# Fused attention and expert layer: DMA issues moved between queues and two pieces of VectorE work reordered

## The chip, the cores and the metric

The kernel runs on one core of one Trainium2 chip. The metric is the device time of one execution in microseconds (us); lower is better. The engines are named PE (TensorE), ACT (ScalarE), DVE (VectorE), POOL (GpSimd) and SP (SyncE).

## The reference

Squared-relu attention in fp32, over 8 batches of 3072 tokens with 256 columns of u and v and 64 columns of z, and then a mixture of 8 experts:

```
scores = (z @ z.T) / S                       # S = 3072, per batch
x      = u * (maximum(scores, 0)**2 @ v)     # rows of all batches, one after the other
logits = x @ w_gate;  e = argmax(logits);  gate = softmax(logits)[e]
# the first `capacity` (768) tokens of each expert are kept, in order; others give 0
out[i] = gate[i] * (maximum(x[i] @ w1[e], 0) @ w2[e])   if i is kept, else 0
```

Once all experts are full, later tokens can't change the output.

## The kernel before

**Arithmetic.** All products run in fp16 with the operands split in a high and a low half, so that each product is three matmuls (high x high, high x low, low x high).

**Groups and pairs.** The attention stage works on groups of 384 queries (three tiles of 128), numbered n = 0, 1, 2, ...; eight groups make a batch (g = n & 7). Group 0 is written out ("peeled"), the others are one loop body per engine (`attention_loop`, L232). A group has 12 steps, one for each pair of key chunks (2 x 128 keys), numbered c = 0 to 11. Work on a pair passes PE (`scores`, L678), ACT (`do_relu` L495, then `do_square` L502), DVE (`do_hi` L1013 casts the fp32 weights to fp16, `do_lo` L1022 takes the rest) and again PE (`weigh`, L731, 18 matmuls). PE does the scores in bursts of three pairs, at c = 0, 3, 6 and 9, each burst three pairs ahead; the burst at c = 9 makes the first three pairs of the next group. ACT runs three pairs ahead of `weigh`, DVE two.

**A finished group.** At c = 11 DVE multiplies the sums with u (`gate_x`, L1056, into ubuf). In the next group, at c = 0, ACT takes row sums of absolute values (l1, L524), DVE makes a power-of-two row scale from them (rscale L1107, rowfac L1110), ACT writes the high halves of the scaled rows (rows_hi, L542) and DVE the low halves (rows_lo, L1117). For each of the three tiles, SP then issues a transposing DMA (xT, L282). PE multiplies xT with the gate weights after tile 1 of c = 3 (logits, L791) and counts the tokens of each expert after tile 1 of c = 4 (counts, L800 and L804). DVE's route at c = 3 takes both: maximum, below, one-hot (up to L1174), then positions from the counts (L1182 to L1189), the flag (`full`, L1191), the softmax sum from ACT's exp (L563; L1195 to L1198) and the slots (L1200 to L1202). POOL scatters the rows to `disp` by slot (L411).

**The end of the stage.** The flag says whether all experts are full. Every engine waits for it and loads it into a register after c = 5 (DVE after c = 4), and does the rest of the group only if the flag allows it (`both_parts`, L248, `load_end`, L241). With these inputs that happens in group n = 18. Then the expert stage follows, 8 experts in halves of 384 rows.

**Queries and keys.** Group n's scores read its 384 queries from q_now (pairs 3 to 11) or q_next (pairs 0 to 2, made in group n - 1), and the first keys of the next batch from k_next. POOL fills these from zP and zQ by DMA within its part of the loop, behind its scatters, when the scores that read the old contents are done (L385 to L398, L424 to L434). PE waits for them at c = 0 and c = 9 (L760 to L769). At c = 5 it also waits, ahead of the flag, for the keys and for the relu that frees the last banks of scores of the group (L762 to L765); `scores` then leaves its own wait for relu_done out in pairs 9 to 11.

**Order of work.** Each engine runs its own instructions in the order in which they are written; semaphores order the engines among each other. `wait_apart` (L218) is a wait on a value in a register, with an increment of a semaphore (`passed`) behind it.

Of the kernel before, what the change touches and what calls it, by code (L numbers as in the profile page):

```python
# [15 lines left out]
I32 = mybir.dt.int32  # L16
# [6 lines left out]
P = 128  # L23
# [23 lines left out]
def relu2_attention_moe(nc, u, v, z, w_gate, w1, w2, out, disp, capacity):  # L47
# [13 lines left out]
    with ExitStack() as ctx:  # L61
# [67 lines left out]
        least = sb("least", [P, 1], F32)  # L129
        full = sb("full", [1, 1], I32)  # L130
        dues = sb("dues", [1, RING], I32)
# [109 lines left out]
        def load_end(eng, n, end):  # L241

            if isinstance(n, int):
                return
            wait_apart(eng, s["flag_ready"], n)
            eng.reg_load(end, full[0:1, 0:1])

# [129 lines left out]
        def _(pool):  # L377
# [3 lines left out]
            pool.partition_all_reduce(amx[:, 1:2], mx[:, 1:2], P, RMAX).then_inc(s["amx0"], 1)  # L381

            def queries(to, m, loaded):

                for key in ("khi_ready", "klo_ready"):  # L385
                    wait_apart(pool, s[key], (m & 126) + 2)
                for q, z16 in zip(to, (zP, zQ)):
                    pool.dma_start(q[:, :], z16[:, bass.ds((m & 15) * GROUP, GROUP)]).then_inc(s[loaded], 16)

            def first_keys(m):  # L390

                for k, z16 in zip(k_next, (zP, zQ)):
                    pool.dma_start(k[:, :], z16[:, bass.ds((m & 8) * (S // 8), SLICE * P)]
                                   ).then_inc(s["loaded_k_next"], 16)

            queries(q_now, 1, "loaded_q_now")
            queries(q_next, 2, "loaded_q_next")
            first_keys(0)  # L398
            pool.wait_ge(s["gmx_ready"], 1)
            pool.partition_all_reduce(gamx[:, :], gmx[:, :], P, RMAX).then_inc(s["gamx_ready"], 1)  # L400

            def body(n, end):
# [21 lines left out]
                def rest():  # L424
                    wait_apart(pool, s["scores_ready"], n * PAIRS + PAIRS)
                    queries(q_now, n + 1, "loaded_q_now")
                    wait_apart(pool, s["scattered"], n * 48)
                    pool.sem_inc(s["row_free"], 1)
                    only_if(pool, g == 3, reduce_maxes)
                    only_if(pool, n == 7, lambda: all_w(0))  # L430
                    only_if(pool, n == 12, lambda: all_w(1))
                    wait_apart(pool, s["scores_ready"], n * PAIRS + PAIRS + BURST)
                    queries(q_next, n + 2, "loaded_q_next")
                    only_if(pool, g == 6, lambda: first_keys(n + 2))  # L434
                only_if(pool, pool.snap(end) > 0, rest)
# [26 lines left out]
        def _(act):  # L462
# [50 lines left out]
            v_hi(UNIT, UNIT)  # L513

            def body(n, end):
                g = n & 7
                peeled = isinstance(n, int)
                K0 = n * PAIRS
                def part(start, stop):
                    for c in range(start, stop):  # L520
# [5 lines left out]
                        if peeled:  # L526
                            if c == 0 or c % BURST:
                                do_relu(K0 + c + 2, c + 2)
                            do_square(K0 + c + 2, c + 2)
                            if c % BURST == 2:  # L530
                                do_relu(K0 + c + 3, c + 3)
                            if c == PAIRS - 1:
                                do_square(K0 + c + 3, c + 3)
                        elif c % BURST == 0:
                            do_relu(K0 + c + 3, c + 3)
                        elif c % BURST == 1:
                            do_relu(K0 + c + 3, c + 3)
                            do_relu(K0 + c + 4, c + 4)
                        if not peeled and c == ROWS_HI_AT:
                            act.wait_ge(s["rscale_ready"], n)  # L540
# [46 lines left out]
                def first_groups(c):  # L587
# [15 lines left out]
                    for q, (group, at) in enumerate(W_HI_IN):  # L603
                        if c == at:
                            only_if(act, n == group, lambda: split_w_hi(0, 0, q))
                both_parts(act, n, end, part)

# [52 lines left out]
        def _(pe):  # L660
# [17 lines left out]
            def scores(K, n, c, par):  # L678


                if not isinstance(K, int):
                    if par is None or c < PAIRS - BURST:
                        wait_apart(pe, s["relu_done"], K - BURST + 1)
                elif K >= BURST:
                    pe.wait_ge(s["relu_done"], K - BURST + 1)
# [40 lines left out]
            def body(n, end, par):  # L726
# [18 lines left out]
                def part(start, stop):  # L745
                    for c in range(start, stop):
                        def burst():
                            first = c + BURST
                            if first < PAIRS:
                                if peeled:  # L750
                                    wait_keys(2 * (first // BURST) + 2, False)
                                for k in range(first, first + BURST):
                                    scores(K0 + k, n, k, par)
# [6 lines left out]
                        if not peeled and c == 0:  # L760
                            wait_apart(pe, s["loaded_q_now"], n * 32)
                        if not peeled and c == END_AT:  # L762

                            wait_keys((n & 120) + 8)
                            wait_apart(pe, s["relu_done"], K0 + PAIRS - BURST)  # L765
                        if not peeled and c == PAIRS - BURST:
# [145 lines left out]
        def _(dve):  # L912
# [161 lines left out]
            def body(n, end):  # L1074
# [21 lines left out]
                def part(start, stop):  # L1096
                    for c in range(start, stop):
# [13 lines left out]
                        if c == PAIRS - 1:  # L1111

                            gate_x(n + 1)
                        if not peeled and c == ROWS_LO_AT:
                            for t in range(TILES):
# [4 lines left out]
                                ins.then_inc(s["rows_lo"], 1)  # L1120
                        do_hi(K0 + c + 2, c + 2, n)
                        do_lo(K0 + c + 2, c + 2)
                        if not peeled and c == DUE_AT:
# [38 lines left out]
                        if not peeled and c == ROUTE_AT[0]:  # L1162
# [12 lines left out]
                                              ).then_inc(s["onehot_ready"], 1)  # L1175
                        if not peeled and c == ROUTE_AT[1]:
                            dve.wait_ge(s["counts_ready"], n)
                            counts = small_counts[:, 0:TILES * E].rearrange("p (t e) -> p t e", t=TILES)

                            def over_tiles(x):  # L1180
# [9 lines left out]
                                                           in1=posf[:, :, :], op0=ALU.mult, op1=ALU.add))  # L1190
                            dve.tensor_scalar(full[0:1, 0:1], least[0:1, :],  # L1191
                                              0.0, float(NG + 1), ALU.is_lt, ALU.mult
                                              ).then_inc(s["flag_ready"], 1)
                            dve.wait_ge(s["exp_ready"], n)
                            route(dve.tensor_reduce(exsum[:, :], ex[:, :, :], AX.X, ALU.add))  # L1195
                            route(dve.scalar_tensor_tensor(out=exsum[:, :], in0=exsum[:, :], scalar=1e-9, in1=rscale[:, :],
                                                           op0=ALU.add, op1=ALU.mult))
                            dve.reciprocal(xrow[:, :, D:D + 1].rearrange("p t a -> p (t a)"), exsum[:, :]  # L1198
                                           ).then_inc(s["slot_ready"], 1)
                            route(dve.tensor_tensor(posf[:, :, :], posf[:, :, :], onehot[:, 0:TILES, :], ALU.mult))  # L1200
# [179 lines left out]
EXP_AT = 4  # L1380
ROUTE_AT = (3, 3)
END_AT = 5
# [12 lines left out]
VLO_AT = (7, 8)  # L1395
ROUTE_STEPS = 2 + 4 + 3 + 2

# [42 lines left out]
```

## Time and profile before

| | |
|---|---|
| median of 3 runs | 860.57 us (860.52 to 860.78) |
| the profiled execution, its own time | 860.57 us |
| its span, first to last instruction | 858.7 us |
| mean granted clock of TensorE | 0.999 of full speed |
| attention stage | to about 602 us |
| expert stage | from there to the end |
| queues | SP and ACT: hardware DMA queue, POOL: software DMA queue |

The profile is of one execution. Times are microseconds from the start of the span. A timeline row gives start, duration, engine, line, operation, output<-input and in brackets the idle time of the engine ahead of it and whose work ended it. The ends of matmuls are modelled: they are pipelined, and neighbours overlap in the record. Register, branch, semaphore and DMA-issuing instructions are not counted as busy.

### The profile page before, as it was taken

How to read it: one execution, taken by the hardware profiler on the slowest of the kernel's cores; microseconds unless marked ns; L12 is line 12 of the kernel's file. 1: busy time of each engine (PE TensorE's matmuls, PEld its weight loads, DVE VectorE, ACT ScalarE, POOL GpSimd, SP SyncE). 2: the span in 40 equal slices, each digit the busy share in tenths (PEclk: the TensorE clock that was granted, in tenths of full speed). 3: DMA queues.
4: the chain of work that ended last, by engine and by line, in shares of the span. 5: the costliest groups of instructions: out<-in, count | busy, mean ns of one | idle time of the engine just before them, and what ended most of it. 6: DMA issues, size and time to landing. Idle time of an engine off the chain costs nothing.

```text
span 858.7 us, 24366 instructions
## 1 busy us (share of the span) xinstructions
PE 835.7 (97%) x7714; PEld 649.0 (76%) x7714; DVE 631.2 (74%) x1360; ACT 561.4 (65%) x873; POOL 167.5 (20%) x198
## 2 busy tenths in 40 slices
PE   6999999999999999999999999999999999999997
PEld 5777777777777777877877877777677777777776
DVE  7977877889889888887888888787555655565521
ACT  7978777768768768776878778578434434435422
POOL 2003202202302211211211320220121221211212
PEclk9999999999999999999999999999999999999999
DMA  8923353343323723313314324722616325415201
GB/s 292 395 72 112 105 171 121 116 155 126 132 58 123 280 82 124 127 49 116 128 49 134 128 62 152 270 71 64 156 46 167 128 62 153 147 43 153 55 18 37
DMA packets 108118, 106.90 MB, mean 124 GB/s; under 512 B 68397, under 2 KB 94202, under 8 KB 107072
## 3 DMA queue, kind: packets, MB, share of 16 engines
q1 hardware_dynamic: 99360, 85.71, 32.2%
q0 software_dynamic: 8736, 20.90, 6.8%
q8 instruction: 13, 0.21, 0.1%
q14 instruction: 9, 0.07, 0.0%
HBM read 40.03 MB, written 44.93 MB: 99 GB/s over the span
## 4 chain that ended last, share of the span: by engine, by line
PE 73%; DVE 12%; issue 9%; DVEq 3%; ACT 2%; POOL 0%; ACTq 0%; POOLq 0%
PE Sc L862 15%; PE O L737 12%; PE O L741 11%; PE O L739 11%; PE Sc L703 9%; DVE attn_hi L1019 4%; PE O L885 3%; PE O L887 3%; PE O L889 3%; DVE attn_lo L1025 2%; ACT xrow L542 2%; PE Sc L885 2%; PE Sc L887 2%; PE Sc L889 2%; DVE ubuf L1066 1%
## 5 line engine op out<-in xcount | busy, mean ns | idle before, releaser
L737 PE MATMUL O<-vS,attn_hi 128*128 128x256 f16 x1332 | 363.9, 273 | 9.9 <-DVE attn_lo L1025 8.5
L741 PE MATMUL O<-vS,attn_lo 128*128 128x256 f16 x1332 | 363.0, 273 | 0.0
L739 PE MATMUL O<-vS,attn_hi 128*128 128x256 f16 x1332 | 363.0, 273 | 0.0
L499 ACT ACTIVATE attn<-Sc 128x768 f32<-128x768 f32 x225 | 172.7, 799 | 100.8 <-DVE attn_lo L1025 63.6
L1025 DVE TENSOR_TENSOR attn_lo<-attn,attn_hi 128x768 f16<-128x768 f32 x223 | 213.7, 958 | 7.7
L504 ACT ACTIVATE attn<-attn 128x768 f32<-128x768 f32 x225 | 185.2, 840 | 3.6 <-ACT xT L474 1.4
L737 PEld LDWEIGHTS O<-vS,attn_hi 128*128 128x128 f16 x1332 | 129.9, 98 | 52.3 <-DVE attn_lo L1025 20.8
L741 PEld LDWEIGHTS O<-vS,attn_lo 128*128 128x128 f16 x1332 | 130.2, 98 | 15.1
L1329 DVE SCALAR_TENSOR_TENSOR rawv<-Sc,rawv 128x768 f16<-128x768 f32 x63 | 60.1, 956 | 110.0 <-ACT rawv L622 64.4
L739 PEld LDWEIGHTS O<-vS,attn_hi 128*128 128x128 f16 x1332 | 130.3, 98 | 13.8
L411 POOL DMA_INDIRECT disp<-xrow,slot x54 | 67.9, 1258 | 366.8 <-DVE slot L1201 355.9
L1019 DVE CAST attn_hi<-attn 128x768 f16<-128x768 f32 x223 | 124.1, 556 | 17.4 <-ACT attn L504 12.7
L622 ACT ACTIVATE rawv<-Sc 128x768 f16<-128x768 f32 x63 | 51.0, 810 | 100.8 <-PE Sc L862 92.8
L703 PE MATMUL Sc<-q_now,zP 64*128 64x384 f16 x477 | 86.7, 324 | 0.1
L703 PE MATMUL Sc<-q_now,zQ 64*128 64x384 f16 x477 | 86.4, 324 | 0.0
L862 PE MATMUL Sc<-vS,w1h 128*128 128x384 f16 x384 | 78.1, 326 | 0.0
L885 PE MATMUL O<-w2s,rawv 128*128 128x256 f16 x256 | 69.8, 273 | 0.0
L889 PE MATMUL O<-w2s,rawv 128*128 128x256 f16 x256 | 69.8, 273 | 0.0
L887 PE MATMUL O<-w2s,rawv 128*128 128x256 f16 x256 | 69.8, 273 | 0.0
L451 POOL DMA_INDIRECT out<-attn,vS x48 | 47.0, 980 | 113.0 <-ACT attn L634 99.8
L703 PEld LDWEIGHTS Sc<-q_now,zP 64*128 64x128 f16 x477 | 40.8, 94 | 25.0 <-issue 11.3
L862 PEld LDWEIGHTS Sc<-vS,w1h 128*128 128x128 f16 x384 | 37.6, 98 | 21.0
(167 smaller groups left out, 1031.5 us busy)
## 6 DMA issues: line engine op xcount, KB each, us to landing
out<-empty SPq DMA_DIRECT2D x16, 1536.0 KB, 5.9
wraw<-in_moe_w SPq DMA_DIRECT2D x16, 1024.0 KB
rawv<-in_v SPq DMA_DIRECT2D x14, 768.0 KB, 7.6
ubuf<-in_u SPq DMA_DIRECT2D x19, 384.0 KB, 3.2
disp<-vS SPq DMA_DIRECT2D x8, 774.0 KB, 11.5
rawz<-in_z SPq DMA_DIRECT2D x3, 768.0 KB
q_now<-zP POOLq DMA_DIRECT2D x18, 96.0 KB, 2.0
q_now<-zQ POOLq DMA_DIRECT2D x18, 96.0 KB, 1.9
```

Of the source, the lines that this page charges most:

```text
L499: act.activation(attn[:, c % BUFS, :, :], Sp[:, score_banks(c), 0:GROUP], ACT.Relu).then_inc(s["relu_done"], 1)
L504: act.activation(attn[:, c % BUFS, :, :], attn[:, c % BUFS, :, :], ACT.Square, scale=ROOT_C).then_inc(s["square_done"], 1)
L703: ins = nc.tensor.matmul(Sp[:, 2 * (c % BURST) + r, 0:GROUP], keys[r], queries[r], start=at == 0, stop=at == len(terms) - 1)
L737: nc.tensor.matmul(o_part(t), hi, v[:, 0:D], start=c == 0 and j == 0 and t % 2 == 0, stop=False, skip_group_check=True)
L739: nc.tensor.matmul(o_part(t), hi, v[:, D:2 * D], start=False, stop=False, skip_group_check=True)
L741: ins = nc.tensor.matmul(o_part(t), lo, v[:, 0:D], start=False, stop=c == PAIRS - 1 and j == 1, skip_group_check=True)
L862: ins = nc.tensor.matmul(Sp[:, 2 * (p % 2) + fi, 0:GROUP], w[par][:, m, f * P:(f + 1) * P], xt[k][:, x + m, :], start=(at == 0), stop=(at ...
L885: nc.tensor.matmul(y_part(t), hi, w2s[:, par, f, 0:D], start=f == 0, stop=False, skip_group_check=True)
L887: nc.tensor.matmul(y_part(t), hi, w2s[:, par, f, D:2 * D], start=False, stop=False, skip_group_check=True)
L889: ins = nc.tensor.matmul(y_part(t), lo, w2s[:, par, f, 0:D], start=False, stop=f == FC - 1, skip_group_check=True)
L1019: dve.tensor_copy(attn_hi[:, b, :, :].rearrange("p j n -> p (j n)"), attn[:, b, :, :].rearrange("p j n -> p (j n)")).then_inc(s["hi_done"], 1)
L1025: dve.tensor_tensor(attn_lo[:, b, :, :], attn[:, b, :, :], attn_hi[:, b, :, :], ALU.subtract).then_inc(s["lo_done"], 1)
```

## The change

Five edits:

1. The DMAs for q_now, q_next and k_next go from POOL's queue to ACT's. ACT issues q_now for the next group at c = 7 (`Q_NOW_AT`) and q_next at c = 10 (`Q_NEXT_AT`), each behind the relus that wait for the scores concerned, and waits for all of them at the end of its group. POOL keeps the scatters and the reductions; its wait for the scatters and the increment of row_free now stand outside the part that depends on the flag.
2. At c = 0 DVE does `do_hi` and `do_lo` (of pair 2) ahead of rows_lo and no longer behind them.
3. In the route, DVE does the softmax sum ahead of the wait for the counts. Since rscale is not folded in any more, the division becomes a reciprocal and a multiplication with rinv: four small instructions in place of three.
4. The flag becomes a ring of four (`ends`), read by an address worked out from n.
5. PE's waits for the keys and for relu_done move from c = 5 to the burst at c = 6, pair by pair, and PE waits for counts_read at c = 6.

```diff
-            eng.reg_load(end, full[0:1, 0:1])
+            eng.reg_load(end, ends[0:1, bass.ds((n - 1) & (RING - 1), 1)])
...
# POOL
-            queries(q_now, 1, "loaded_q_now")
-            queries(q_next, 2, "loaded_q_next")
-            first_keys(0)
...
                 def rest():
-                    wait_apart(pool, s["scores_ready"], n * PAIRS + PAIRS)
-                    queries(q_now, n + 1, "loaded_q_now")
-                    wait_apart(pool, s["scattered"], n * 48)
-                    pool.sem_inc(s["row_free"], 1)
                     only_if(pool, g == 3, reduce_maxes)
                     only_if(pool, n == 7, lambda: all_w(0))
                     only_if(pool, n == 12, lambda: all_w(1))
-                    wait_apart(pool, s["scores_ready"], n * PAIRS + PAIRS + BURST)
-                    queries(q_next, n + 2, "loaded_q_next")
-                    only_if(pool, g == 6, lambda: first_keys(n + 2))
+                wait_apart(pool, s["scattered"], n * 48)
+                pool.sem_inc(s["row_free"], 1)
...
# ACT
+            def queries(to, m, loaded):
+                for q, z16 in zip(to, (zP, zQ)):
+                    act.dma_start(q[:, :], z16[:, bass.ds((m & 15) * GROUP, GROUP)]).then_inc(s[loaded], 16)
+            def first_keys(m):
+                for k, z16 in zip(k_next, (zP, zQ)):
+                    act.dma_start(k[:, :], z16[:, bass.ds((m & 8) * (S // 8), SLICE * P)]
+                                  ).then_inc(s["loaded_k_next"], 16)
+            def keys_split(m):
+                for key in ("khi_ready", "klo_ready"):
+                    wait_apart(act, s[key], (m & 126) + 2)
...
                         elif c % BURST == 1:
                             do_relu(K0 + c + 3, c + 3)
                             do_relu(K0 + c + 4, c + 4)
+                        if c == Q_NOW_AT:
+                            keys_split(n + 1)
+                            queries(q_now, n + 1, "loaded_q_now")
+                            if peeled:
+                                first_keys(0)
+                        if c == Q_NEXT_AT:
+                            keys_split(n + 2)
+                            queries(q_next, n + 2, "loaded_q_next")
+                            if not peeled:
+                                only_if(act, g == 6, lambda: first_keys(n + 2))
...
-                both_parts(act, n, end, part)
+                def part_and_copies(start, stop):
+                    part(start, stop)
+                    if stop == PAIRS:
+                        wait_apart(act, s["loaded_q_now"], n * 32 + 32)
+                        wait_apart(act, s["loaded_q_next"], n * 32 + 32)
+                        wait_apart(act, s["loaded_k_next"], ((n + 2) & 120) * 4 + 32)
+                both_parts(act, n, end, part_and_copies)
...
# PE
-                    if par is None or c < PAIRS - BURST:
-                        wait_apart(pe, s["relu_done"], K - BURST + 1)
+                    wait_apart(pe, s["relu_done"], K - BURST + 1)
...
+                                elif first == PAIRS - BURST:
+                                    wait_keys((n & 120) + 8)
...
-                        if not peeled and c == END_AT:
-                            wait_keys((n & 120) + 8)
-                            wait_apart(pe, s["relu_done"], K0 + PAIRS - BURST)
+                        if not peeled and c == PAIRS - 2 * BURST:
+                            wait_apart(pe, s["counts_read"], n)
...
# DVE
+                        do_hi(K0 + c + 2, c + 2, n)
+                        do_lo(K0 + c + 2, c + 2)
                         if not peeled and c == ROWS_LO_AT:
                             for t in range(TILES):
...
-                        do_hi(K0 + c + 2, c + 2, n)
-                        do_lo(K0 + c + 2, c + 2)
...
                         if not peeled and c == ROUTE_AT[1]:
+                            dve.wait_ge(s["exp_ready"], n)
+                            route(dve.tensor_reduce(exsum[:, :], ex[:, :, :], AX.X, ALU.add))
+                            route(dve.tensor_scalar(exsum[:, :], exsum[:, :], 1e-9, None, ALU.add))
+                            route(dve.reciprocal(exsum[:, :], exsum[:, :]))
+                            dve.tensor_tensor(xrow[:, :, D:D + 1].rearrange("p t a -> p (t a)"), exsum[:, :], rinv[:, :],
+                                              ALU.mult).then_inc(s["slot_ready"], 1)
+                        if not peeled and c == ROUTE_AT[2]:
                             dve.wait_ge(s["counts_ready"], n)
...
-                            dve.tensor_scalar(full[0:1, 0:1], least[0:1, :],
+                            dve.tensor_scalar(ends[0:1, bass.ds((n - 1) & (RING - 1), 1)], least[0:1, :],
                                               0.0, float(NG + 1), ALU.is_lt, ALU.mult
                                               ).then_inc(s["flag_ready"], 1)
-                            dve.wait_ge(s["exp_ready"], n)
-                            route(dve.tensor_reduce(exsum[:, :], ex[:, :, :], AX.X, ALU.add))
-                            route(dve.scalar_tensor_tensor(out=exsum[:, :], in0=exsum[:, :], scalar=1e-9, in1=rscale[:, :],
-                                                           op0=ALU.add, op1=ALU.mult))
-                            dve.reciprocal(xrow[:, :, D:D + 1].rearrange("p t a -> p (t a)"), exsum[:, :]
-                                           ).then_inc(s["slot_ready"], 1)
...
-ROUTE_AT = (3, 3)
+Q_NOW_AT = 7
+Q_NEXT_AT = 10
+ROUTE_AT = (3, 3, 3)
```

## Rows read from the trace of the kernel before

**Rows 1.** Page, part 1: busy us, share of the span, instructions.

```profile
PE 835.7 (97%) x7714; PEld 649.0 (76%) x7714; DVE 631.2 (74%) x1360; ACT 561.4 (65%) x873; POOL 167.5 (20%) x198
```

**Rows 2.** Waits of PE: who waited for whom, us in total, times, longest.

```profile
PE O L737 <- DVE attn_lo L1025: 8.5, 18, 1.2
```

**Rows 3.** Timeline of PE, group 9: start, us, [idle before <-releaser].

```profile
302.69 0.33 PE L703 MATMUL Sc<-q_now,zP 64*128 64x384 f16 x1
...
308.68 0.28 PE L737 MATMUL O<-vS,attn_hi 128*128 128x256 f16 x1 [0.32 <-DVE attn_lo L1025]
...
310.75 0.33 PE L703 MATMUL Sc<-q_now,zP 64*128 64x384 f16 x1
...
313.64 0.45 PE L791 MATMUL Sc<-wgs,xT 128*128 128x16 f16 x12
...
318.72 0.33 PE L703 MATMUL Sc<-q_now,zP 64*128 64x384 f16 x1
...
326.29 1.64 PE L703 MATMUL Sc<-q_next,k_next 64*128 64x384 f16 x18
```

**Rows 4.** Timeline of DVE, group 9.

```profile
305.13 0.17 DVE L1107 TENSOR_SCALAR rscale<-rinv 128x3 int32<-128x3 int32 x1
...
305.87 1.28 DVE L1117 SCALAR_TENSOR_TENSOR xrow<-ubuf,rscale,xrow 128x256 f16<-128x256 f32 x3 [0.45 <-ACT xrow L542]
...
307.66 0.96 DVE L1025 TENSOR_TENSOR attn_lo<-attn,attn_hi 128x768 f16<-128x768 f32 x1
...
316.19 0.16 DVE L1182 TENSOR_TENSOR base<-base,Sc 128x8 f32<-128x8 f32 x1 [0.66 <-PE Sc L804]
...
317.06 0.14 DVE L1191 TENSOR_SCALAR full<-least 1x1 int32<-1x1 f32 x1
...
318.55 0.96 DVE L1025 TENSOR_TENSOR attn_lo<-attn,attn_hi 128x768 f16<-128x768 f32 x1
319.43 0.56 DVE L1019 CAST attn_hi<-attn 128x768 f16<-128x768 f32 x1
```

**Rows 5.** Timeline of ACT, group 9.

```profile
302.92 0.42 ACT L524 ACTIVATE xrow<-ubuf 128x256 f16<-128x256 f32 x1 [1.41 <-DVE ubuf L1066]
...
315.32 0.22 ACT L563 ACTIVATE ex<-logit 128x24 f32<-128x24 f32 x1
```

**Rows 6.** Timelines of SP and ACT; DMA issues (KB each, median us to landing).

```profile
306.46 3.97 SPq L282 DMA_TRANSPOSE xT<-xrow  x3
...
xT<-xrow SPq DMA_TRANSPOSE x54, 2.4
...
0.71 0.88 SPq L261 DMA_DIRECT2D rawz<-in_z  x2
...
rawz<-in_z SPq DMA_DIRECT2D x2, 384.0 KB, 3.5
...
3.96 1.79 ACT L468 ACTIVATE attn<-rawz 128x768 bf16<-128x768 f32 x2 [1.75 <-DMA rawz<-in_z]
```

**Rows 7.** DMA issues on POOL (groups by line: busy us, mean ns) and SP.

```profile
L388 POOL DMA_DIRECT2D q_now<-zP x18 | 12.2, 680 | 0.0
...
310.70 0.37 SPq L283 DMA_DIRECT2D ubuf<-in_u  x1
```

**Rows 8.** Timelines of DVE and PE, group 8.

```profile
273.96 0.17 DVE L1107 TENSOR_SCALAR rscale<-rinv 128x3 int32<-128x3 int32 x1
...
277.50 0.28 PE L737 MATMUL O<-vS,attn_hi 128*128 128x256 f16 x1 [1.18 <-DVE attn_lo L1025]
...
282.46 0.45 PE L791 MATMUL Sc<-wgs,xT 128*128 128x16 f16 x12
```

**Rows 9.** Timelines of DVE and PE, group 11.

```profile
390.07 0.55 DVE L1255 TENSOR_REDUCE mx<-Sc 128x1 f32<-128x384 f32 x1
...
391.44 1.64 PE L703 MATMUL Sc<-q_next,k_next 64*128 64x384 f16 x18 [1.55 <-DVE mx L1255]
```

**Rows 10.** Timeline of PE, the close of group 18.

```profile
601.99 0.49 PE L819 MATMUL O<-vS,attn_hi 128*128 128x256 f16 x3
```

More of the change, by code:

```diff
@@ L129, in relu2_attention_moe @@
         least = sb("least", [P, 1], F32)
-        full = sb("full", [1, 1], I32)
+        ends = sb("ends", [1, RING], I32)
         dues = sb("dues", [1, RING], I32)
@@ L381, in _ @@
             pool.partition_all_reduce(amx[:, 1:2], mx[:, 1:2], P, RMAX).then_inc(s["amx0"], 1)
[L383 to L394, printed above, removed]
-            queries(q_now, 1, "loaded_q_now")
-            queries(q_next, 2, "loaded_q_next")
-            first_keys(0)
             pool.wait_ge(s["gmx_ready"], 1)
@@ L1395 @@
 VLO_AT = (7, 8)
-ROUTE_STEPS = 2 + 4 + 3 + 2
+ROUTE_STEPS = 2 + 2 + 2 + 4 + 2
 _INS = ['u', 'v', 'z', 'moe_w_gate', 'moe_w1', 'moe_w2']
```

## The prediction

> **What bounds the kernel now.** I read the engines' shares first: TensorE (PE) is busy for 97% of the span [rows 1]. So time can only come from the places where PE stands still. The waits of PE say where [rows 2]: nearly all its idle time is one kind, 18 waits for attn_lo of VectorE (DVE), 8.5 us in the model of the trace, one in each attention group n = 1 to 18. The expert stage (from 602 us) has none worth naming and the change doesn't touch it. Then I read PE's timeline over group n = 9 [rows 3]. Score bursts start at 302.69, 310.75, 318.72 and 326.29: pitches of 8.06, 7.97 and 7.57 us. 7.57 is three pairs of chunks with nothing between. The second pitch has the logits and counts matmuls in it (0.40, real work). The first is 0.49 too long, and that is the wait at 308.68, which the trace prints as 0.32. It understates each such wait by 0.17, since the modelled end of a matmul overlaps the next one. So the loss is 8.5 + 18 x 0.17 = 11.6 us, 1.3% of the run, and no more than that can be had here, but for one wait in group 11 (below).
>
> **The stall and its release (do_hi/do_lo ahead of rows_lo).** In group 9, DVE has written rowfac and then waits 0.45 us for ACT's xrow, from 305.42 to 305.87, does the three rows_lo (1.28), and only then the hi and lo of pair 2, whose lo runs from 307.66 to 308.62; PE starts at 308.68 [rows 3, 4]. The square of that pair belongs to the group before, so its data lie ready. The two take 1.47 together (308.62 less the end of rows_lo, 305.87 + 1.28 = 307.15). Put first, hi starts at 305.42 and lo ends at 306.89. PE wants it at 308.68 - 0.49 = 308.19: 1.3 us to spare. In group 8, where the wait was longest (1.18 printed, 1.35 real), rscale starts at 273.96, two small steps (0.29, from the same steps in group 9: 305.42 less 305.13) and 1.47 bring lo's end to 275.72, and PE wants it at 277.50 - 1.35 = 276.15 [rows 4, 8]. Still early. All 18 waits go: **-11.6 us**.
>
> What is late next: pair 3's hi starts when rows_lo end, 306.89 + 1.28 = 308.2, lo ends 309.7, and PE wants pair 3 after the burst and pair 2, at 310.26 + 1.6 = 311.9. Fine.
>
> The price is that rows_lo move back by the 1.47 less the 0.45 of waiting: 1.02. Behind them is SyncE: three transposes, issued back to back in 3.97 us from 306.46, 2.4 us to landing [rows 6]. The last starts at about 306.46 + 2.71 = 309.17 and lands at 311.6; PE wants it at 313.64, a slack of 2.0. After the change it lands at 312.6 and PE comes at 313.15: slack 0.55. In group 8 PE comes 1.35 earlier: 282.46 - 1.35 = 281.11 [rows 8]; the same chain counted from rscale (309.17 + 2.4 + 1.02 - 305.13 = 7.4) gives 281.4, less 0.35 for the shorter route (next part) 281.05. That is level. Five groups have waits of the long kind, 5 to 8 and 10 (the longest, 8, is shown), and are near this; bounds for them 0 to 0.4 us each. I take **+0.3 us** in all.
>
> **The route on DVE.** Now DVE waits 0.66 us for the counts [rows 4] and later does three steps on exsum. Those go into the wait, as four (the division is now a reciprocal and a multiply). They need exp: ACT's exp ends at 315.54 [rows 5], onehot at 316.19 - 0.66 = 315.53, so the new wait for exp is 0.05 at most. Four small steps of 0.15 (six steps from 316.19 to 317.06) to 0.2 each are 0.6 to 0.8: the flag comes between 0.1 earlier and 0.2 later against PE than before, and the end of the route is some 0.35 earlier (0.66 less one more step, less the exp wait). It gains only where DVE is late afterwards: PE's wait of 1.55 for mx in group 11 [rows 9], **-0.35 us**.
>
> **Queries and keys issued by ACT and no longer by POOL.** Per group four plain DMAs, two at pair 7 and two at pair 10, and two more in groups 0, 6 and 14. No row shows one on ACT. POOL's take 0.68 us to issue (by software), SyncE's plain load 0.37 [rows 7]. Bounds 0 and 0.68, I take 0.4, nearest to SyncE's: 1.6 us on ACT per group. Behind them in ACT's queue stand square 10 and squares 13 and 14. ACT is busy for 65% of the span and idles 1.41 ahead of a group's l1 [rows 1, 5]; these squares are one pair ahead of DVE, so I expect that nothing reaches PE. POOL loses four waits and the DMAs and only has the scatter left: no gain, nobody waited for it. The new waits of ACT at the end of a group, for q_now, q_next and k_next: the last is issued some 2.5 us before ACT's idle time ends and takes 2.4 by the old queue, so it hides in the 1.41. Where a weight split stands at pair 10 (groups 8, 9) up to 0.8 us of it may push l1, and then the transposes, once or twice. Group 0 keeps ACT full and takes six issues. **+0.3 us** (0 to 1.5).
>
> **PE's own queue at pair 6.** The waits for relu_done and for the keys move from pair 5, ahead of the flag's load and branch, to the burst behind them, and counts_read and a ring address are added. The semaphores themselves are all set early: relu 8 stands ahead of the exp of 315.32 in ACT's queue and the counts are read before the flag of 317.06, against a burst at 318.72. What may cost is the queue's walk: flag written by 317.20, burst at 318.72, so 1.52 us [rows 3, 4], about 1.35 to 1.5 after the change. Load and branch take at most 0.88 (DVE does both, with two more waits, between lo 6 at 318.55 and hi 7 at 319.43 without idle), and on PE at the last group's turn they show no gap at all [rows 4, 10]. In group 11, mx ends at 390.62 and the burst starts at 391.44: 0.82 for leaving a branch and about five waits with their increments [rows 9]. Five waits more and the address are then 0.3 to 0.8. Sum 0.9 to 1.6 against 1.35 to 1.5: bounds 0 to 0.25 us in each of 17 groups, 0 to 4 us. I take **0**, since most of 0.88 is probably DVE's two other waits.
>
> This needs PE's queue to run ahead of its array by over a microsecond, and in the last group it runs ahead by at least the load and branch. The Trainium skill (Advanced Engine Details and Errata, Engine Queue Depths) gives TensorE a queue of 64 entries and VectorE and ScalarE one of 8. By that rule PE has some 30 matmuls in hand, and the walk is hidden as far as the flag allows: 0 us; with a short queue it would be the upper bound. The gapless close of the last group agrees with the rule as far as it goes.
>
> **Sum.** The profiled run took 860.57 us (span 858.7 and 1.9 around it), which is also the median. 860.57 - 11.6 - 0.35 + 0.3 + 0.3 = **849.2 us**.
>
> **Rivals.**
> A. *The queue walk at pair 6 shows.* For it: everything moved there sits behind a load and a branch. Against: now the pitch up to that burst is 7.57 and the 0.40 of real work, so load and branch cost nothing there [rows 3]. 17 x 0.15 to 0.45 = 2.5 to 7.5 us: about **854 us**.
> B. *The transposes become the wait (slower).* If a landing time counts from the issue's end and not from its start, the last one lands 1.2 later: 313.8 in group 9, and PE, due at 313.15, waits 0.7. 13 groups of 0.7 and 5 of about 1.2 are 15.1 us: **864 us**. It decides from a landing 0.55 us later than I reckon. Against: the first loads were issued at 0.71, take 3.5 to landing and ACT starts on the first at 3.96, which fits only a count from the start [rows 6].
> C. *A DMA issue holds ACT for far longer,* say until it lands (2 us). Then squares come 4 us late where they are at most some 2 ahead of need, and PE stands 2 us in each group: 849.2 + 2 x 18 = **885 us**. Against: POOL and SyncE issue in 0.7 and 0.4 [rows 7].
> D. *The stall comes back one step later,* half of it, because DVE, busy for 74% of the span [rows 1] and fuller in the groups that also split keys, values or weights, can't follow a faster PE: **855 us**. Against: the long waits are in 5 groups only, and the change frees 0.8 us of DVE per group (0.45 and 0.35). If instead nothing at all is gained, 860.6.
>
> **Chances.** Forecast 0.68, A 0.14, B 0.07, C 0.03, D 0.08 (of it 0.04 with no gain). This kernel's change is told from none at about 0.2%, 1.7 us. Faster: 0.68 + 0.14 + 0.04 = 0.86; same 0.04; slower 0.10. The forecast's own range is 847.5 to 851.5; with A and the better half of D the range is 847 to 857, which leaves out some 0.17.
>
> **What would show it.** Right: PE's waits for attn_lo gone (under 1 us in all), the first pitch of a group 7.6 and the group's period 30.7 us; DVE without the 0.45 before xrow and the 0.66 before base; the last transpose landing about 0.5 before the logits; ACT's DMA issues at 0.3 to 0.5 each. A: the gap ahead of the pair-6 burst over 0.21. B: PE or DVE waiting for xT at the logits, a second pitch over 7.97. C: ACT idle after its DMAs and the squares late. D: waits for attn_lo left in groups 5 to 8.

## The result and the profile after

The changed kernel takes 868.49 us (median of 4 runs, 867.05 to 870.21) against 860.67 before: the ratio is 1.0091, 95% interval 1.007 to 1.0111, so it is **slower by 0.9%**. I had forecast 849.2. The profiled execution took 866.55 us (span 864.8).

First the waits of PE in the changed kernel (who waited for whom, us in total, times, longest), to be read against [rows 2]:

```profile
PE Sc L712 <- issue: 8.5, 19, 0.7
...
PE Sc L800 <- DMA xT<-xrow: 3.8, 6, 0.7
PE O L746 <- DVE attn_lo L1034: 2.2, 4, 0.7
```

The wait for attn_lo (8.5 us before) is down to 2.2, and two new ones stand in its place: score bursts (L712) late by "issue", which is PE's own queue with nothing else to blame, and logits (L800) that wait for the transposes. PE's timeline in group 14 of the changed kernel answers to [rows 3]:

```profile
466.51 0.33 PE L712 MATMUL Sc<-q_now,zP 64*128 64x384 f16 x1
...
474.08 0.33 PE L712 MATMUL Sc<-q_now,zP 64*128 64x384 f16 x1
...
482.55 0.32 PE L712 MATMUL Sc<-q_now,zP 64*128 64x384 f16 x1 [0.43 <-issue]
...
490.12 1.64 PE L712 MATMUL Sc<-q_next,k_next 64*128 64x384 f16 x18
```

Pitches are the distances from one burst's start to the next. Here they are 7.57, 8.47, 7.57: the first is as short as forecast (8.06 before), the second is 0.50 over its 7.97. Where the time is, over groups 1 to 18, as the excess of each pitch over 7.57, 7.97, 7.57 and 7.57 us, summed from the burst starts in the two traces:

| us | before | after |
|---|---|---|
| start of group 0 | 21.32 | 21.59 |
| group 0 beyond 28.32 | 0.0 | 1.4 |
| first pitch (waits for attn_lo) | 11.7 | 3.5 |
| second pitch (waits for xT, burst at pair 6) | 0.0 | 12.5 |
| third pitch (norms in groups 3 and 11) | 3.5 | 2.7 |
| fourth pitch | 0.1 | 0.2 |
| group 18 after its pair-3 burst | 0.0 | 0.75 |

The differences add up to 5.9 us, and the attention stage ends 5.9 us later (closing matmuls at 607.93 and 601.99 [rows 10]). The timed runs of the changed kernel are 0.5 to 3.7 us above the profiled one, which this table doesn't explain.

DVE does as planned. In group 14, rows_lo (L1128) start without the wait of 0.45 [rows 4], and the counts (L1199) find no wait of 0.66. But the flag comes late:

```profile
470.72 1.27 DVE L1128 SCALAR_TENSOR_TENSOR xrow<-ubuf,rscale,xrow 128x256 f16<-128x256 f32 x3
...
479.60 0.15 DVE L1199 TENSOR_TENSOR base<-base,Sc 128x8 f32<-128x8 f32 x1
...
480.26 0.17 DVE L1206 SCALAR_TENSOR_TENSOR posf<-fullp,posf 128x24 f32<-128x24 f32 x1
480.56 0.14 DVE L1208 TENSOR_SCALAR ends<-least 1x1 f32 x1
```

The flag (L1208) ends at 480.70, 6.62 us after the pair-3 burst, where it was 6.45 in group 9 before (317.20 - 310.75 [rows 3, 4]). From the flag's end to the burst at 482.55 are 1.85 us; the text calls this stretch the walk of PE's queue.

ACT's timeline at the end of group 9 and the start of group 10 has the DMA issues (ACTq):

```profile
335.94 1.51 ACT L477 ACTIVATE attn<-Sc 128x768 f32<-128x768 f32 x2 [0.29 <-ACT xT L452]
336.66 0.49 ACTq L496 DMA_DIRECT2D q_next<-zP  x1
337.25 0.56 ACTq L496 DMA_DIRECT2D q_next<-zQ  x1
338.01 0.84 ACT L482 ACTIVATE attn<-attn 128x768 f32<-128x768 f32 x1 [0.55 <-ACT attn L477]
338.76 1.13 ACT L622 ACTIVATE w2s<-wraw,wscale 128x1024 f16<-128x1024 f32 x1
339.80 0.83 ACT L482 ACTIVATE attn<-attn 128x768 f32<-128x768 f32 x1
340.53 0.40 ACT L518 ACTIVATE xrow<-ubuf 128x256 f16<-128x256 f32 x1
```

An issue takes 0.49 to 0.56 us and the next 0.1 more to begin. The pair runs beside the second relu and leaves ACT idle for 0.55 ahead of the square. The l1 (L518) starts 2.62 us after PE's burst at 337.91, and 1.24 after it (335.10 against 333.86) in the kernel before.

Group 9 begins late for another reason. Here ACT stands still before the l1, and what it waits for is the landing of q_next:

```profile
301.13 0.85 ACTq L496 DMA_DIRECT2D q_next<-zQ  x1
...
307.78 0.42 ACT L518 ACTIVATE xrow<-ubuf 128x256 f16<-128x256 f32 x1 [2.98 <-DMA q_next<-zQ]
```

This DMA landed 5.8 us after its issue, where most take 1.9 to 2.0.

### The profile page after: what moved, and what is told of

The parts are those of the page before. It is cut to its first block, busy times and chain, and to the rows that moved or that the text cites. A ratio compares the mean times of both kernels' runs of the same rounds, so it can differ in the third digit from the quotient of the medians.

```text
span 864.8 us, 24723 instructions
## 1 busy us (share of the span) xinstructions
PE 836.9 (97%) x7714; PEld 652.5 (75%) x7715; DVE 636.4 (74%) x1379; ACT 564.6 (65%) x874; POOL 123.3 (14%) x121
## 4 chain that ended last, share of the span: by engine, by line
PE 75%; issue 8%; ACT 6%; DMA 3%; ACTq 3%; DVE 2%; SPq 2%; DVEq 0%; POOL 0%; POOLq 0%
PE Sc L871 14%; PE O L746 12%; PE O L748 12%; PE O L750 12%; PE Sc L712 9%; PE O L894 3%; PE O L898 3%; PE O L896 3%; ACT attn L477 3%; PE Sc L898 2%; PE Sc L896 2%; PE Sc L894 2%; SPq L282 1%; DMA xT<-xrow 1%; ACTq L496 1%
## 5 line engine op out<-in xcount | busy, mean ns | idle before, releaser
L712 PE MATMUL Sc<-q_now,zP 64*128 64x384 f16 x477 | 86.8, 323 | 7.4 <-issue 7.3
L712 PE MATMUL Sc<-q_now,zQ 64*128 64x384 f16 x477 | 86.1, 324 | 0.0
L712 PEld LDWEIGHTS Sc<-q_now,zP 64*128 64x128 f16 x477 | 41.0, 94 | 32.0 <-issue 19.3
```

Source lines behind the costliest of these rows:

```text
L712: ins = nc.tensor.matmul(Sp[:, 2 * (c % BURST) + r, 0:GROUP], keys[r], queries[r], start=at == 0, stop=at == len(terms) - 1)
```

## The experiments

All ratios are to the kernel before on the same chip. "Second pitch" is that of the ordinary groups: not group 1, and not the groups in which PE waits for xT.

**lo_first: edit 2 alone.** The kernel before with

```diff
+                        do_hi(K0 + c + 2, c + 2, n)
+                        do_lo(K0 + c + 2, c + 2)
                         if not peeled and c == ROWS_LO_AT:
...
-                        do_hi(K0 + c + 2, c + 2, n)
-                        do_lo(K0 + c + 2, c + 2)
```

> The kernel before with edit 2 alone (hi and lo of pair 2 ahead of rows_lo). Theory: the 18 waits of PE for attn_lo go, 11.6 us of real loss, and nothing new comes, since flag, PE's waits and ACT's queue are as before: 849 us, the first pitch of a group 7.57. Rival (the transposes, moved back by a microsecond, become the wait): PE waits for xT at the logits in most groups, second pitch over 8.1, and the time stays over 855 us.

Measured 850.28 us, ratio 0.9876 (0.9862 to 0.9891). The first pitch is 7.57 in all 18 groups. The second is 7.97 but in groups 5 to 8 and 10, where it is up to 0.52 (group 8) longer, 1.1 us in all: the waits for xT that I had put at 0.3. The forecast's step on the stall holds, and the rival doesn't show: with rows_lo moved back, the other groups stay at 7.97.

**undo_pe: the change without edit 5; undo_act: without edit 1; only_pe: the kernel before with edit 5.** The edits are those of the diff above, taken back or applied alone.

> The changed kernel with edit 5 undone: PE's waits for keys and relu_done are at pair 5 again, ahead of the flag, and counts_read isn't waited for. Theory (the walk of PE's queue from flag to burst is too long by the added waits): the second pitch goes from 8.48 to about 7.97 in 17 groups, 9 us less, about 859.5 us; what ACT's DMA issues cost stays. Rival (the flag itself is late, or its load from a ring is slow): the second pitch stays over 8.3 and the time over 865 us.

Measured 857.61 us, ratio 0.9966 (0.9953 to 0.9978). Second pitch 7.97 again, with the flag as late as in the change (6.62). Group 9's first pitch is 7.57 here, without an edit that bears on it.

> The changed kernel with edit 1 undone: q_now, q_next and k_next are issued by POOL again. Theory (ACT's issues of 0.5 us delay its queue in group 0 and, beside other work, the l1 of groups 2, 3, 9, 10, 11 and 18): group 0 loses its 1.37 us, no wait for attn_lo is left, the waits for xT go, about 8 us less, 860 us, with the second pitch 8.48 in all groups. Rival (those waits come from DVE's new order alone): they stay, and the time is over 866 us.

Measured 857.59 us, ratio 0.9964 (0.9951 to 0.9977). All first pitches 7.57, group 0 at its 28.3, no wait for xT; second pitch 8.43 to 8.51. The stage ends at 598.89 and not 607.93: ACT's part of the loss is 9.0 us in the profiles.

> The kernel before with edit 5 alone (PE's waits behind the flag, counts_read waited for). Theory (the waits alone are the cost): second pitch up by 0.3 to 0.5 us in 17 groups, 866 to 869 us. Rival (only a later flag or the ring's load makes the walk too long): the second pitch stays 7.97 and the time 860.6 us, and the walk has slack for five more waits.

Measured 861.67 us, ratio 1.0012 (1.0003 to 1.0021). My theory failed here: second pitch 8.01, hardly longer. The waits alone are nearly hidden, though taking them out of the changed kernel saves all of its 0.5. So several edits must share one slack.

**undo_ring: the change without edit 4.**

> The changed kernel with edit 4 undone (one flag at a fixed address). The runs so far read as: burst at pair 6 = flag's end + walk of PE's queue, where the flag ends 6.45 us after the burst at pair 3 (6.62 in the changed kernel) and the walk is 1.55 with PE's waits behind the flag and 1.85 with the ring as well. Theory (the ring's address costs 0.30 in the walk and 0.09 on DVE ahead of the flag): second pitch 6.53 + 1.55 = 8.08 and not 8.48, 17 x 0.40 = 6.8 us less, about 861.7 us. Rival (the walk depends on when the flag comes, not on the ring): second pitch over 8.3, time over 865.5 us.

Measured 859.24 us, ratio 0.9982 (0.997 to 0.9995). Second pitch 8.07 to 8.13 for 8.08 forecast; the flag ends at 6.54 and the walk is 1.55. The saving is 9.3 us by the medians, larger than the 6.8 I named: groups 0 and 9 came out better in this profile too. For group 9 the traces show the reason. The last copy of q_next in group 8 landed 2.0 to 2.1 us after its issue here and in undo_pe, and 5.8 in the changed kernel. For group 0 (0.6 us) the reason stays open.

**flag_late: the walk by itself.** The kernel before, with the flag written later:

```diff
-                            dve.tensor_scalar(full[0:1, 0:1], least[0:1, :],
-                                              0.0, float(NG + 1), ALU.is_lt, ALU.mult
-                                              ).then_inc(s["flag_ready"], 1)
...
                             dve.tensor_copy(base[:, 0, :], base[:, 1, :])
+                            dve.tensor_scalar(full[0:1, 0:1], least[0:1, :],
+                                              0.0, float(NG + 1), ALU.is_lt, ALU.mult
+                                              ).then_inc(s["flag_ready"], 1)
```

> The kernel before, with the step that writes the flag moved behind the rest of the route (five small steps, some 0.9 us later); nothing else. It measures how long PE's queue walks from the flag to the burst at pair 6 when nothing but the load and the branch is there. Theory (load and branch 0.8, the moved waits 0.75, the ring 0.3, which add up to the 1.85 seen): flag ends 7.35 after the burst at pair 3, so the second pitch is 8.15. Rival (load and branch alone take the 1.34 that the runs so far allow, and the waits only 0.2): 8.7.

Measured 864.67 us, in a single run, so that the reading rests on its timeline and not on its time. DVE's and PE's timelines of group 13, whose pair-3 burst is at 441.22 (flag, then burst):

```profile
448.39 0.14 DVE L1200 TENSOR_SCALAR full<-least 1x1 int32<-1x1 f32 x1
...
449.31 0.33 PE L703 MATMUL Sc<-q_now,zP 64*128 64x384 f16 x1
```

The flag ends at 448.53, the burst starts 0.78 later; second pitch 8.09. It is 0.77 to 0.82 in groups 2 to 17. So PE takes 0.79 us from the flag over load and branch to the first matmul.

**ring_pe: edits 4 and 5 on the kernel before.**

> The kernel before with edits 4 and 5 (ring and PE's waits), the rest as before. Theory (flag's end + walk): the flag ends at 6.54 (the ring's address on DVE is 0.09), the walk is 1.85, second pitch 8.39 in 17 groups, 7 us more than before, 868 us. Rival (it takes the new route as well): 7.97 to 8.05, 861 to 862 us.

Measured 866.9 us, ratio 1.0066 (1.0048 to 1.0084). The timelines of group 13, pair-3 burst at 442.56:

```profile
448.97 0.14 DVE L1190 TENSOR_SCALAR ends<-least 1x1 f32 x1
...
450.97 0.32 PE L702 MATMUL Sc<-q_now,zP 64*128 64x384 f16 x1 [0.37 <-issue]
```

Flag's end at 449.11 is 6.55, the walk 1.86, the pitch 8.41 for 8.39 forecast. So one formula gives the second pitch in the ordinary groups of every kernel here: the greater of 7.97 and flag's end + walk.

| kernel | flag's end | walk | sum | measured |
|---|---|---|---|---|
| before | 6.45 | 0.79 (load, branch) | 7.24 | 7.97 |
| flag_late | 7.29 | 0.79 | 8.08 | 8.06 to 8.11 |
| only_pe | 6.45 | 1.55 (+0.76, PE's waits) | 8.00 | 7.98 to 8.03 |
| undo_ring | 6.54 | 1.55 | 8.09 | 8.07 to 8.13 |
| ring_pe | 6.54 | 1.85 (+0.30, ring's address) | 8.39 | 8.37 to 8.44 |
| after, undo_act | 6.62 | 1.85 | 8.47 | 8.43 to 8.51 |
| undo_pe | 6.62 | at most 1.34 | below 7.97 | 7.97 |

0.79 was measured by flag_late; 0.76 and 0.30 are differences between the other rows. In group 1 the walk is 0.2 to 0.3 longer in each of them. Where PE waits for xT, DVE's route and the flag come late too, and the walk stays as it is: in groups 2, 3, 9, 10 and 11 of the changed kernel the flag ends at 7.33 to 7.38, the walk is 1.83 to 1.88, and the pitches are 9.17 to 9.26. The burst follows the flag wherever it comes, at a constant distance. This speaks against the relu or the keys as the late wait; and counts_read is set 0.9 us ahead of the flag's end (group 14).

**only_act: edit 1 alone on the kernel before.**

> The kernel before with edit 1 alone (queries and keys issued by ACT). Theory (two issues of 0.5 us put 0.4 to 0.5 us into ACT's queue twice a group, and l1 comes late where ACT has sums or a weight split at pairs 6 to 10): 1.4 us in group 0 and about 1.4 in each of groups 2, 3, 9, 10, 11 and 18, whose first pitch goes to 9 or more, other groups as before: about 870 us. Rival (it costs only with DVE's new order, through xT): 862 us or less.

Measured 876.53 us, ratio 1.0173 (1.0156 to 1.019), worse than I expected: first pitches of 11.06, 11.08, 10.52 and 11.44 in groups 2, 3, 9 and 10, and 9.1 to 9.5 in groups 11, 17 and 18. ACT's timeline at the start of group 2 has idle time ahead of the l1 (L518), where the kernel before has none:

```profile
81.64 0.56 ACTq L496 DMA_DIRECT2D q_next<-zQ  x1
82.40 1.58 ACT L482 ACTIVATE attn<-attn 128x768 f32<-128x768 f32 x2 [0.58 <-ACT attn L477]
84.54 0.42 ACT L518 ACTIVATE xrow<-ubuf 128x256 f16<-128x256 f32 x1 [0.56 <-issue]
```

The DMA at 81.64 landed at 83.64, and the l1 starts 0.90 later. This distance is 0.84 to 0.91 in groups 2, 3, 9, 11, 17 and 18 of this run and in groups 2, 3, 9, 11 and 18 of the changed kernel. So ACT waits for the landing, and its queue then needs some 0.9 us more to the l1. In groups 9 and 17 of this run the landings took 5.5 and 4.8 us.

PE then stands 2.24 us at pair 2, from 87.6 to 89.84. What comes on top shows in two stretches of the windows (from:to, us, busy of PE, PEld, DVE, ACT, POOL, PEclk, DMA share, GB/s):

```profile
86.00:90.00 4.00, 1.76 (x17) 1.33 (x16) 3.45 (x10) 4.00 (x8) 0.00 (x0) 1.00 0.16 33
90.00:94.00 4.00, 4.00 (x26) 2.48 (x26) 3.52 (x8) 1.39 (x2) 0.00 (x0) 0.59 0.57 141
```

After that stall the granted clock is 0.59 on average over 4 us, so for most of them at 1.2 GHz and not at 2.4: 26 matmuls there, and 39 and 41 in stretches of 4 us ahead of the stall. Taken from the excess of the first two pitches, less the stall, the slow clock costs 1.6 us in each of groups 2, 3, 9 and 10, beside stalls of 2.1 to 2.5 us (0.17 more than printed). In groups 11, 17 and 18 PE stands 1.5 to 1.95 us, the clock stays at 1.00, and nothing comes on top.

**wait_later: the change, with ACT's waits moved into the next group.**

```diff
-                    if stop == PAIRS:
-                        wait_apart(act, s["loaded_q_now"], n * 32 + 32)
-                        wait_apart(act, s["loaded_q_next"], n * 32 + 32)
-                        wait_apart(act, s["loaded_k_next"], ((n + 2) & 120) * 4 + 32)
+                    if start == 0 and not isinstance(n, int):
+                        wait_apart(act, s["loaded_q_now"], n * 32)
+                        wait_apart(act, s["loaded_q_next"], n * 32)
+                        wait_apart(act, s["loaded_k_next"], ((n + 1) & 120) * 4 + 32)
```

> The changed kernel, with ACT's waits for q_now, q_next and k_next at the first part of the next group, ahead of the flag, where ACT idles over 3 us, and not at the end of its group. Theory (issue time is the cost): the late groups stay late but for one where ACT waited 3 us for a landing, 866 to 868.5 us. Rival (the wait for the landing holds l1 back): groups 2, 3, 9, 10, 11 and 18 lose their long first pitch, about 861 us.

Measured 862.52 us, ratio 1.0015 (1.0006 to 1.0025): 6 us less than the change, between the two theories. The first pitches are 7.57 again in groups 3, 9, 11 and 18, and the sum of their excess falls from 3.5 to 0.75; the waits for xT fall from 3.8 us to 2.2 and stay in groups 2, 3, 10, 11 and 18. Both the wait for the landing and the issues cost. The wait is 6.0 of ACT's 10.9 us by the medians. In the profiles it is 4.5 of 7.9 us over groups 1 to 18, and only 3.5 of 9.0 over the whole stage, since group 0 and what stands ahead of it took 1.0 us longer here, without a reason that I can show. Which part is the larger isn't settled.

**q_now_act: edits 2 and 3, and q_now alone on ACT** (its two DMAs at pair 7, its wait at the end of the group; q_next and k_next on POOL).

> Edits 2 and 3 (849.0 us), and only q_now issued by ACT, at pair 7, with its wait at the end of the group; q_next and k_next stay with POOL. Its landing is over well before the group ends, so only the issues count. Theory (1.15 us of issues, 0.4 to 0.7 us of delay to l1 in the groups with sums): group 0 loses 0 to 0.5, and groups 2, 3, 10, 11 and 18 wait 0.1 to 0.3 for xT each: 850 to 851 us. Rival (issues are free, only the wait for q_next's landing costs): 849 us with no wait for xT.

Measured 849.58 us, ratio 0.9862 (0.9847 to 0.9877). One wait for xT is left (group 10, 0.6), group 0 loses nothing. q_now on ACT is all but free, with the second pitch's slack still there. By difference, what costs is q_next, issued at pair 10 and waited for at once, and in group 0 also the keys; no run has these alone.

**lo_route: edits 2 and 3 alone.**

> The kernel before with edits 2 and 3 alone. Theory: as with edit 2 alone (850.3 us), and the shorter route takes away what is left of waits for xT in groups 5 to 8 and 10 (1.1 us) and 0.35 us in each of groups 3 and 11: 848.7 us. The flag comes 0.08 later, which the walk of 1.34 or less hides. Rival (the later flag shows, or exp comes late): second pitch over 7.97 in most groups, 850.5 us or more.

Measured 848.96 us, ratio 0.9857 (0.9841 to 0.9874). Groups 5 to 7 are at 7.97, groups 8 and 10 keep 0.11 and 0.17, the norms' pitch in group 11 goes from 9.81 to 9.41, and the later flag (6.53) is hidden, as the formula says (6.53 + 0.79 is less than 7.97).

**norm_first: the same, with the norms' maximum ahead of hi and lo at pair 8.**

```diff
+                        if not peeled and c == NRM_AT:
+                            def next_norm():
+                                wait_apart(dve, s["nrm_psum"], (n & 120) + 8)
+                                dve.tensor_reduce(mx[:, 0:1], norm_sums, AX.X, ALU.max).then_inc(s["nrm_done"], 8)
+                            only_if(dve, g == 3, next_norm)
                         do_hi(K0 + c + 2, c + 2, n)
                         do_lo(K0 + c + 2, c + 2)
```

> Edits 2 and 3 (849.0 us), and DVE's maximum of the norms in groups 3 and 11 ahead of the hi and lo of its step, for which PE waits before the burst at pair 9. Theory (PE's wait goes, as the norms are ready when DVE gets there): third pitch 8.2 and not 8.83 and 9.41, 1.8 us less, 847.2 us. Rival (DVE then waits for PE's norms, or is late for pair 10): no gain, 849 us or more.

Measured 847.31 us, ratio 0.9837 (0.9823 to 0.9851), the best kernel of the study, 2.4% below the changed one by the medians. In group 11 the maximum is done at 380.82 and the burst starts at 381.79 without a wait (1.55 us before [rows 9]):

```profile
380.26 0.56 DVE L1117 TENSOR_REDUCE mx<-Sc 128x1 f32<-128x384 f32 x1
...
381.79 1.64 PE L703 MATMUL Sc<-q_next,k_next 64*128 64x384 f16 x18
```

## Why the prediction was wrong

**The stall and its release: right.** Edit 2 alone gives 10.6 us (860.91 to 850.28), the 18 losses of 11.6 less 1.1 of waits for xT. In the step "The price is that rows_lo move back" the mechanism and the groups were right and the term was 0.3 where lo_first has 1.1, and with the shorter route 0.3 (lo_route).

**The route on DVE: right in size.** 0.4 us in group 11 for 0.35 forecast, and edits 2 and 3 together are at 848.96, beside the forecast of the whole.

**"PE's own queue at pair 6 ... I take 0": the first step that failed.** I had the mechanism (rival A), and the window right: 1.35 us were left, of 1.35 to 1.5 named. The walk was mis-sized. Load and branch 0.79 was within my 0.88, but I took "most of 0.88" to be DVE's two other waits, and it wasn't. The waits and the ring's address are 1.06, where I had 0.3 to 0.8. I had these from 0.82 us in group 11 "for leaving a branch and about five waits". By the kernel's text three waits stand there between the one for mx and the first matmul, so that each is dearer than I took it, and edit 5 puts four ahead of the burst's first matmul, not five. Sum 1.85 against 1.35: 0.5 in each of 17 groups, 8.8 us in undo_act's second pitches. My upper bound of 0.25 was the arithmetic of 1.6 against 1.35; rival A went up to 0.45, against the same rows. Three edits that each are hidden alone (0.03 for the waits, nothing for the flag's 0.08 or for a ring without the waits, in undo_pe) spent one slack of 0.73 (7.97 - 7.24) together: 0.17 on the flag and 1.06 on the walk, 0.50 more than there was. The flag was the limit, since flag's end + walk fits the pitches of all ordinary groups that are longer than 7.97. The Trainium skill (Advanced Engine Details and Errata, Engine Queue Depths) gives TensorE a queue of 64 entries. By that rule alone I expected the pitch to stay at 7.97; it is 8.47, so depth doesn't hide a walk that begins only at the flag. No run here measures the depth itself.

**"Queries and keys issued by ACT ... +0.3 us": the second.** It measured 9.0 us in the profiles (undo_act against the change), 10.9 by the medians. An issue takes 0.49 to 0.56 and not 0.4, which is small. The failure is the cover. I took the 1.41 us of idle time ahead of one group's l1 for all groups. ACT has none at the end of groups 1, 2, 9, 10 and 17, where it also takes sums or splits a weight at pairs 6 to 10, as the end of group 9 shows (the next l1 at 335.10, right behind a square). There the issues and the landing of a DMA that is issued at pair 10 go straight into l1, rows_lo and the transposes. The sixth, at the end of group 8, was bad luck: it has the 1.41, but I reckoned with a landing of 2.4 us, and it took 5.8. That is 1.6 us in the pitches of group 9, which undo_pe and undo_ring don't have. And the transposes had lost their slack to edit 2: six groups wait for xT, 0.6 to 0.7 each, where only_act, without edit 2, has no such wait. Rival B had this place and another reason; lo_first's ordinary groups at 7.97 fit a landing counted from the issue, as I said, and the transposes are late because ACT is.

Part of this was the wait for attn_lo again, 0.3 to 0.8 in the first pitch of the same six groups. By the medians the two failed terms fill the gap: from 848.96 us (lo_route, edits 2 and 3) edits 4 and 5 lead to 857.59 (undo_act), 8.6 more, and edit 1 to 868.49, another 10.9. That is 19.5 us, and 19.3 lie between the forecast of 849.2 and the result.

## What to carry to other kernels

Where several edits put work behind the same event, add up the whole queue from that event to the first instruction that matters, before and after, against one slack: the parts may each be free and the sum not. Measure such a slack by delaying the event on purpose, as flag_late does. For work given to an engine "with idle time", look for the iteration in which it has none, and let nothing wait for a transfer's typical landing time where its longest one doesn't fit.

## What the runs showed of the hardware

A wait on a register's value with its increment, a load with an address worked out from a register, and a branch are not free on PE's queue: load and branch 0.79 us, the moved and added waits 0.76 (four of them stand ahead of the first matmul), the address 0.30 more on PE and 0.09 on DVE (480.26 to 480.56 in place of 0.21). None of it is counted as busy; it shows as "issue".

A plain DMA of 96 KB issued by ACT takes 0.49 to 0.56 us (0.54 on POOL at best in the kernel before) and overlaps only with the instruction already running. It lands after 1.9 to 2.0 us in the median and after up to 5.9 in the changed kernel (groups 8 and 16). In group 0 the first issue for k_next (192 KB) took 1.18.

In only_act four PE stalls, printed as 1.97 to 2.31 us, were each followed by a stretch at 1.2 GHz (granted clock 0.50 over 2 us, as in 92:94) that cost 1.6 us. Three of 1.34 to 1.78 us were followed by none (1.00). In the changed kernel, whose longest wait of PE in groups 1 to 18 is 0.7 us, the stretches of 2 us behind the waits of groups 2, 9 and 18 are all at 1.00.
